# Attention and MoE in one stream: two slices side by side on TensorE, x moved to another PSUM bank, its scaling one step later

## What is computed

```python
scores = (q @ k.T) / sqrt(64)               # 2 batches, 8 heads, 576 tokens, head size 64
kth    = 32nd largest of each row of scores
attn   = softmax(where(scores >= kth, scores, -1e9))
x      = (attn @ v) as 1152 tokens x 512
h      = x @ w_in                           # 512 -> 2048
x2     = (h * sigmoid(h)) @ w_out           # 2048 -> 512
P      = exp(x2 @ w_gate - max); 8 rounds: rows to 1, columns to 144
out    = sum over 8 experts e of P[:, e] * (relu(x2 @ w1[e]) @ w2[e])
```

## Time and profile before

| | |
|---|---|
| Median of 3 runs | 1322.34 us (1320.54 to 1323.52) |
| The profiled execution | 1318.93 us, its span 1317.1 us |
| Busy over the span | TensorE 96%, VectorE 50%, ScalarE 35%, GpSimd 28% |
| Granted TensorE clock | 1.000 (mean over the span) |
| First stage | 0 to about 508 us |

### The profile page before, as it was taken

The page is one execution under the profiler, slowest core; times in us unless marked ns, Lnnn a source line. Parts: engine busy times, 40 slices in busy tenths (PEclk is TensorE's granted clock), DMA queues, the critical chain, the costliest instruction groups (busy, mean ns, idle before and its releaser), DMA issues.

```text
span 1317.1 us, 21296 instructions
## 1 busy us (share of the span) xinstructions
PE 1262.9 (96%) x8109; PEld 1117.0 (85%) x8109; DVE 664.9 (50%) x1485; ACT 456.9 (35%) x960; POOL 365.8 (28%) x321
## 2 busy tenths in 40 slices
PE   6888999999999999999999999999999999999999
PEld 4677787877777899898898898898898998998997
DVE  5999999999999326422222222222222222222222
ACT  3666766667667333021121121121120220220210
POOL 2665434434343422031131131130230230330300
PEclk9999999999999999999999999999999999999999
DMA  5863746636535542120120120110110110210001
GB/s 142 287 214 122 270 158 222 220 97 225 201 120 223 229 194 96 32 64 19 46 64 13 51 64 0 64 64 0 64 64 0 64 61 3 64 49 15 0 0 72
DMA packets 72929, 130.14 MB, mean 99 GB/s; under 512 B 42016, under 2 KB 42016, under 8 KB 63648
## 3 DMA queue, kind: packets, MB, share of 16 engines
q1 hardware_dynamic: 72864, 129.27, 28.6%
HBM read 110.12 MB, written 19.14 MB: 98 GB/s over the span
## 4 chain that ended last, share of the span: by engine, by line
PE 77%; DVE 13%; POOL 5%; ACT 3%; issue 2%; DMA 0%; SPq 0%; ACTq 0%
PE banks L409 24%; PE banks L411 23%; PE banks L410 23%; DVE stats L862 5%; DVE rest L873 5%; POOL probs L1110 2%; POOL wd_lo L1088 2%; PE banks L477 1%; POOL wu_lo L1088 1%; PE banks L444 1%; DVE g_f L926 1%; PE banks L453 1%; PE banks L470 1%; ACT scores L685 1%; ACT wu_hi L761 1%
## 5 line engine op out<-in xcount | busy, mean ns | idle before, releaser
L822 ACT ACTIVATE h_hi<-banks 128x384 fp32r<-128x384 f32 x192 | 94.5, 492 | 624.5 <-PE banks L411 624.5
L409 PE MATMUL banks<-x_lo,wu_hi 128*128 128x384 f32 x768 | 257.3, 335 | 0.0
L411 PE MATMUL banks<-x_hi,wu_hi 128*128 128x384 f32 x768 | 256.8, 334 | 0.0
L410 PE MATMUL banks<-x_hi,wu_lo 128*128 128x384 f32 x768 | 256.6, 334 | 0.0
L1088 POOL TENSOR_TENSOR wu_lo<-wu_raw,wu_hi 128x512 fp32r<-128x512 f32 x76 | 95.8, 1288 | 559.2 <-ACT wu_hi L761 552.3
L987 DVE SCALAR_TENSOR_TENSOR h_lo<-banks,h_hi 128x384 fp32r<-128x384 f32 x192 | 106.7, 557 | 281.7 <-ACT h_hi L822 281.7
L1029 DVE SCALAR_TENSOR_TENSOR y_acc<-banks,plan_e,y_acc 128x512 f32<-128x512 f32 x135 | 101.4, 751 | 272.3 <-PE banks L411 272.3
L409 PE MATMUL banks<-wd_lo,h_hi 128*128 128x512 f32 x576 | 227.2, 394 | 0.0
L411 PE MATMUL banks<-wd_hi,h_hi 128*128 128x512 f32 x576 | 227.0, 394 | 0.0
L410 PE MATMUL banks<-wd_hi,h_lo 128*128 128x512 f32 x576 | 227.0, 394 | 0.0
L862 DVE MAX8 stats<-rest 128x8 f32<-128x576 f32 x216 | 155.9, 748 | 0.1
(11 more groups left out here) (104 smaller groups left out, 1805.1 us busy)
## 6 DMA issues: line engine op xcount, KB each, us to landing
wu_raw<-in_moe_w_dram SPq DMA_DIRECT2D x32, 512.0 KB, 3.7
wd_raw<-in_moe_w_dram SPq DMA_DIRECT2D x32, 512.0 KB, 3.7
wu_hi<-kept_up_hi SPq DMA_DIRECT2D x14, 1024.0 KB, 5.9
wu_lo<-kept_up_lo SPq DMA_DIRECT2D x14, 1024.0 KB, 8.7
wd_hi<-kept_down_hi SPq DMA_DIRECT2D x14, 1024.0 KB, 6.0
wd_lo<-kept_down_lo SPq DMA_DIRECT2D x14, 1024.0 KB, 8.6
q_nat<-in_q_dram SPq DMA_DIRECT2D x64, 72.0 KB, 2.2
wu_raw<-in_moe_w_in_dram SPq DMA_DIRECT2D x8, 512.0 KB, 4.9
```

The costliest lines, as they stand in the source:

```text
L409: pe.matmul(to, a_hi, b_lo, start=first, stop=False)
L410: pe.matmul(to, a_lo, b_hi, start=False, stop=False)
L411: return pe.matmul(to, a_hi, b_hi, start=False, stop=last)
L822: act.activation(h_hi[:, f, CH * c:CH * (c + 1)], ps_up[:, at % UBANKS, 0:CH], ACT.Relu).then_inc(h_hi_done, 1)
```

## The change

- TensorE's step is reordered. Before: slice 0, weigh values, scores, spread, slice 1, transposes of probabilities, transposes of a head. After: scores, spread (of the tile one step older), slice 0, slice 1, weigh values, transposes of probabilities, transposes of a head.
- x of a unit moves from the second bank of `ps_t` to the bank of K transposed. `transpose_probs` no longer waits for its copy; `weigh_values` waits for the copies of K and Q, and the transposes of K wait for the copied x.
- The sums are spread and x is scaled one step later; their reciprocals get a second pair of columns.
- `least_kept` scales its two columns with two one-input `tensor_scalar` instead of one two-input `tensor_tensor` with a constant tile.
- The slices begin 5 steps behind the attention instead of 4, and everything tied to them shifts by one step. `keep_clock` gives 12 products a step instead of 10.
- ScalarE copies scores earlier in its step, and both split pieces come ahead of the penalty.

```diff
-FIRST_SLICE = 4
+FIRST_SLICE = 5
-STEPS = range(ALL + NT + 5)
+STEPS = range(ALL + NT + 6)
-        XO, RO = P, QT
+        XO, RO = QT, QT
+        def reciprocal_of(tile):
+            at = 36 + tile // 2 % 2
+            return stats[:, tile % 2, at:at + 1]
...
-            def transpose_head(hh, spread):
+            def transpose_head(hh, spread, weighed):
...
                 need(pe, x_scaled, spread)
                 if hh // H % 2 == 0:
+                    need(pe, o_copied, weighed)
...
             def transpose_probs(tile):
...
-                need(pe, o_copied, units_by(tile - 1))
...
             def weigh_values(tile):
...
                 pe.wait_ge(pT_copied, tile + 1)
+                pe.wait_ge(kq_ready, heads_by(tile + 4))
...
-                            last = pe.matmul(ps_t[D * j:D * (j + 1), 1, XO:XO + P],
+                            last = pe.matmul(ps_kq[D * j:D * (j + 1), 0, XO:XO + P],
...
             def spread_sums(tile):
...
-                pe.wait_ge(kq_ready, heads_by(tile + 4))
+                pe.wait_ge(kq_ready, heads_by(tile + 5))
...
             for step in STEPS:
+                if step + 1 < ALL:
+                    scores_of(step + 1)
+                if 0 <= step - 4 < ALL:
+                    spread_sums(step - 4)
                 silu_slice(slice_at(step, 0))
                 if step < NT + FIRST_SLICE:
-                    keep_clock(ps_m[:, 1, 0:P], 4)
-                if 0 <= step - 3 < ALL:
-                    weigh_values(step - 3)
-                if step + 1 < ALL:
-                    scores_of(step + 1)
-                if 0 <= step - 3 < ALL:
-                    spread_sums(step - 3)
+                    keep_clock(ps_m[:, 1, 0:P], 6)
...
                 silu_slice(slice_at(step, 1))
                 if step < NT + FIRST_SLICE:
                     keep_clock(ps_m[:, 1, 0:P], 6)
+                if 0 <= step - 3 < ALL:
+                    weigh_values(step - 3)
                 if 0 <= step - 2 < ALL:
                     transpose_probs(step - 2)
-                transpose_head(head_at(step + 2), units_by(step - 3))
+                transpose_head(head_at(step + 2), units_by(step - 4), units_by(step - 3))
```

ScalarE's step, where `copy_scores` and `copy_output` move:

```diff
                 if 0 <= step - 3 < ALL:
                     copy_pT(step - 3)
+                if step + 1 < ALL:
+                    copy_scores(step + 1)
                 g_high(slice_at(step - 1, 0))
...
                 g_high(slice_at(step - 1, 1))
-                if 0 <= step - 3 < ALL:
-                    copy_output(step - 3)
-                if step + 1 < ALL:
-                    copy_scores(step + 1)
                 split_pieces(pieces_at(step, 0))
+                split_pieces(pieces_at(step, 1))
                 if 0 <= step - 1 < ALL:
                     penalise(step - 1)
-                split_pieces(pieces_at(step, 1))
                 take_slice(slice_at(step, 1))
+                if 0 <= step - 3 < ALL:
+                    copy_output(step - 3)
                 copy_kq(head_at(step + 2))
```

VectorE's step, and the biases:

```diff
-                dve.tensor_tensor(st[:, 32:34], st[:, 0:TOPK:TOPK - 1], factors[:, :], ALU.mult).then_inc(kth_ready, 1)
+                dve.tensor_scalar(st[:, 32:33], st[:, 0:1], -(D ** -0.5), None, ALU.mult)
+                dve.tensor_scalar(st[:, 33:34], st[:, TOPK - 1:TOPK], PENALTY, None, ALU.mult).then_inc(kth_ready, 1)
...
                 if old:
                     search(step - 1, 2)
+                if 0 <= step - 3 < ALL:
+                    guard_sum(step - 3)
                 if new:
                     search(step, 0)
...
                 if old:
                     least_kept(step - 1)
+                if 0 <= step - 4 < ALL:
+                    scale_output(step - 4)
                 if new:
                     remove(step, 1)
                 take_slice(slice_at(step, 0))
-                if 0 <= step - 2 < ALL:
-                    guard_sum(step - 2)
-                if 0 <= step - 3 < ALL:
-                    scale_output(step - 3)
```

More of the change, by code:

```diff
@@ L500, in spread_sums @@
                         last = pe.matmul(ps_kq[D * j:D * (j + 1), 1, RO:RO + P],
-                                         stats[:, (tile - 1 + j) % 2, 35:36].to_broadcast([P, D]), ident[:, :],
+                                         reciprocal_of(tile - 1 + j).to_broadcast([P, D]), ident[:, :],
                                          start=True, stop=True)
@@ L791, in _ @@
                     copy_pT(step - 3)
+                if step + 1 < ALL:
+                    copy_scores(step + 1)
                 g_high(slice_at(step - 1, 0))
-                if step % NT == 3 and NT <= step < ALL + NT:
+                if step % NT == 4 and NT <= step < ALL + NT:
                     split_output(step // NT - 1, 2)
@@ L798, in _ @@
                 g_high(slice_at(step - 1, 1))
+                split_pieces(pieces_at(step, 0))
+                split_pieces(pieces_at(step, 1))
+                if 0 <= step - 1 < ALL:
+                    penalise(step - 1)
+                take_slice(slice_at(step, 1))
                 if 0 <= step - 3 < ALL:
                     copy_output(step - 3)
-                if step + 1 < ALL:
-                    copy_scores(step + 1)
-                split_pieces(pieces_at(step, 0))
-                if 0 <= step - 1 < ALL:
-                    penalise(step - 1)
-                split_pieces(pieces_at(step, 1))
-                take_slice(slice_at(step, 1))
                 copy_kq(head_at(step + 2))
-                if step % NT == 17 and step < ALL:
-                    split_output(step // NT, 0)
-                if step % NT == 6 and 2 * NT < step < ALL:
+                if step % NT == 0 and 0 < step < ALL + NT:
+                    split_output(step // NT - 1, 0)
+                if step % NT == 7 and 2 * NT < step < ALL:
                     sums_high(step // NT - 2)
@@ L886, in guard_sum @@
                 dve.wait_ge(exp_done, tile + 1)
-                dve.tensor_scalar(st[:, 36:37], st[:, 34:35], 1e-9, None, ALU.add).then_inc(guarded, 1)
+                dve.tensor_scalar(st[:, 35:36], st[:, 34:35], 1e-9, None, ALU.add).then_inc(guarded, 1)
             def invert_sum(tile):
@@ L891, in invert_sum @@
                 dve.wait_ge(guarded, tile + 1)
-                dve.reciprocal(st[:, 35:36], st[:, 36:37]).then_inc(rinv_ready, 1)
+                dve.reciprocal(reciprocal_of(tile), st[:, 35:36]).then_inc(rinv_ready, 1)
             def scale_output(tile):
@@ L947, in _ @@
                               ALU.subtract).then_inc(gate_split, 1)
-            dve.wait_ge(made, 6)
+            dve.wait_ge(made, 4)
             for step in STEPS:
@@ L978, in _ @@
                     split_pieces(pieces_at(step, 1))
-                if step == ALL + 6:
+                if step == ALL + 7:
                     split_sums(QUARTERS - 2, slice(0, KD))
@@ L1128, in _ @@
                     split_pieces(pieces_at(step, 1))
-                if step % NT == 0 and 0 < step < ALL + NT:
+                if step % NT == 1 and 1 < step < ALL + NT:
                     output_lows(step // NT - 1, 0)
-                if step % NT in (7, 8) and 2 * NT < step < ALL:
-                    sums_low(step // NT - 2, step % NT - 7)
+                if step % NT in (8, 9) and 2 * NT < step < ALL:
+                    sums_low(step // NT - 2, step % NT - 8)
             pool.wait_ge(lane_max, 1)
```

25 lines of the change are left out of this document (11 added, 14 removed).

## The result

The changed kernel takes 1338.5 us (median of 4 runs, 1337.2 to 1339.0) against 1322.3 us. The ratio is 1.0124 with a 95% interval of 1.0112 to 1.0136: slower by 16 us, where the prediction said 1322.5 us and at most 1334. The profiled execution has a span of 1335.4 us, 18.3 us more than before.

The account below looks back on a forecast made before the run. VectorE was taken nearly to set the pace of the attention steps, TensorE little behind; stretch sums of -2.7 us plus 3.2 for coupling gave +0.5 on the profiled 1318.9, which lies 3.4 under the median: 1322.5 us, range 1309 to 1334.

Parts of the forecast that it names:

- The one-input biases: VectorE's 32nd-score scaling: 12.7 us of excess from GpSimd's lock goes, the pair costs 1.4 us, net gain 11.3 us.
- rival (d): VectorE's scaling: one-input operations keep the lock, so that part does nothing: +2 to +3 us, 1325; chance 0.06.
- The head's stall: TensorE before scores: waits for ScalarE's copies of a head just transposed, 0.96 or 0.66 us each, 24.0 us for 30.
- rival (c): Head's copies come late on ScalarE, 1.72 us a head; TensorE bounds everywhere: +10 to +20 us, 1332 to 1342; chance 0.22.
- rival (b): Attention steps: VectorE is the only bound, TensorE's stalls fall into slack: -16.8 us, 1305.5, halfway 1314; chance 0.22.
- the sum as the greater of two ledgers: Attention stretches: each takes the longer of TensorE's and VectorE's work; the stretches and the tail sum to -2.7 us.
- The half of 6.5 us allowed for coupling: Three slice stretches: today they exceed the greater ledger by 6.5 us in all; 3.2 us added to the forecast.
- The early stretch: 22 to 118 us: TensorE 91.6, VectorE 83 of 96 us, so -4.4 us; with the five steps after it, -0.7.
- Fillers: TensorE, 23 steps ahead of the slices: 112 more filler instructions at 0.12 us, 13.4 us, 9 of them in the stretches.
- Slices later: End of attention: one step's slices, 1.78 at 1.59 us, move from under VectorE to behind it, +2.8 us.
- The pair's saving: TensorE: a second slice directly behind the first takes 1.59 instead of 1.77 us, 0.18 a pair, 2.5 us a quarter.

Follow-up runs that it names:

- a_early: Changed kernel with K and Q of a head transposed, copied and loaded one step earlier: 1324.2 us, ratio 1.002 to the kernel before.
- a_act: Changed kernel with ScalarE's copy of scores back behind the exponential and the high parts: 1335.4 us, ratio 1.0103 to the kernel before.
- a_early_act: Changed kernel with heads transposed one step earlier and ScalarE's copy of scores back behind the exponential: 1318.2 us, ratio 0.9968 to the kernel before.
- b_bias: Kernel before with only the two biases made by one-input operations: 1317.6 us, ratio 0.9966.
- b_late: Kernel before with only the slices and all tied to them one step later: 1316.5 us, ratio 0.996.
- a_early_act_ring: Changed kernel with heads one step earlier, scores' copy behind the high parts, and high parts of weights first on ScalarE: 1310.7 us, ratio 0.9918 to kernel before.
- b_all: Kernel before with one-input biases, high parts of weights ahead of the exponential, and slices one step later: 1304.8 us, ratio 0.9879.
- b_bias_ring: Kernel before with one-input biases and the high parts of both weight pieces ahead of the exponential on ScalarE: 1308.7 us, ratio 0.9895.
- a_fill10: Changed kernel with 10 filler products a step instead of 12 in the 23 steps ahead of the first slice: 1339.5 us, ratio 1.0139 to kernel before.
- a_two: Changed kernel with the two biases from one two-input operation again: 1342.3 us, ratio 1.0148 to the kernel before.
- a_ring_fill10: Changed kernel with high parts ahead of the scores' copy and the exponential, and 10 filler products a step: 1327.7 us, ratio 1.005 to kernel before.

## Why the prediction was wrong, step by step

**The one-input biases: right in size, wrong in effect.** The excess of 12.7 us went away in full, at no price for the pair (0.02 us a step was booked). The Trainium skill (SBUF, "Who interferes with whom") says that a one-input tensor_scalar can enter a two-port mode and contend with GpSimd as well, if its operands meet that mode's conditions. For one column nothing of it shows: 138 instructions in the groups above average 0.144 and 0.135 us; rival (d) is out. But 11.3 us on an engine is not 11.3 us at the end: undone or done alone it is 3.8 and 4.1 us. 7.7 of the 12.7 us (0.43 x 18) lay in the early steps, where the ring took them.

**The head's stall: right.** 24.0 us were booked for 30 heads, 25.4 measured, and ScalarE was prompt: the mean wait at scores is 14.2/23 = 0.62 us in the later quarters, as forecast (0.4 to 0.7). In the early stretch it is 6.4 us in 7 waits, 0.91 each, above the forecast but under the 1.1 us that would have meant rival (c). That rival had the right sign and its time range, 1332 to 1342, holds the result; its mechanism, late copies at 1.72 us a head, did not take place, so its hit is luck. (In rival (b), 18 steps at 5.2 us against 104.6 make -11.0 and not -10.7 us; nothing hangs on it.)

**The step that failed: the sum as the greater of two ledgers.** It let a stall on TensorE vanish wherever VectorE's ledger was as long. Quarter 2 shows it. TensorE's ledger there said 105.1 us, of which 7.7 were head stalls, 97.4 without. Read from start to start in the trace, the 18 steps take 111.3 us between transposes of P, 14.9 of them stalls, 96.4 without. The work and the head stalls (7.2) are as booked. Not booked are the other 7.7 us: 4.2 at the first slice behind scores (a slice starts 2.22 instead of 1.70 us before the next in the mean of 8, the low part's wait), 2.3 from the transposes of P to what follows (0.67 instead of 0.54 us), 1.2 in second slices (1.67 instead of the booked 1.59). With all of them TensorE's ledger is the greater one wherever slices run, VectorE's idle time is 31 us where 20 were forecast, and the greater part of each stall is paid: taking the heads' 25.4 us away gives 14.4 us, and behind tile 22's mark 11.2 of 16.0. It is not all of it, and the parts don't simply add: in quarter 2 the heads' 7.2 us give back 3.8 alone (a_early), the scores' copy alone gives nothing (112.1 us still, a_act), and the two together 7.4 (104.7 us, a_early_act). The half of 6.5 us allowed for coupling had no ground in a mechanism.

**A wait that was not listed.** The diff moves `copy_scores` ahead of the high parts. The prediction names the move and prices only ScalarE's promptness for K and Q. What the moved instruction itself waits for (GpSimd's subtraction), and what is then queued behind it, was not asked. TensorE's waits for low parts are 9.2 us from 118 to 440 us, before 2.4; moving the copy back takes 4.8 of them away, worth 3.1 us alone and 6.0 once the heads are out of the way. The other 4.4 us stay without the move. The longest of them (1.39 us, at 289.07 in a_act) is GpSimd's own queue: the high part is ready at 286.66, but GpSimd makes the low part of x from 285.37 (1.42 us) and then a subtraction (1.42 us), and starts on the slice's low part only at 288.12. The subtraction at 141.63 in the earlier trace rows held a hint: it had itself waited 3.66 us for ScalarE, so its end, for which the copy waits, could come late.

**The early stretch: a third bound.** Forecast -0.7 us, measured +0.9. Both ledgers (91.6 and 83 us for 96) were under the time that the stretch took, and 4.4 us were booked as gain. The gap was not slack but the ring of ScalarE and GpSimd at 5.95 us a step. The 93.3 busy us that made VectorE look like the bound held some 7 us of stretched multiplies: with them gone it is 86.45 us at the same pace (b_bias). The ring stood in the trace of before, in ScalarE's list of waits from 20 to 118 us, of which the prediction makes nothing:
```profile
ACT probs L697 <- POOL probs L1110: 31.5, 16, 2.7
```
16 waits in 16 steps, 2 us each, is what this ring looks like. In the changed kernel the same wait has another name, since the copy of scores now comes first (its list, same stretch):
```profile
ACT scores L690 <- POOL probs L1114: 26.8, 16, 2.9
```
The ring also takes rival (b) down: VectorE alone would have given 5.2 us a step there, and only kernels with the ring cut come near that pace.

**Fillers.** The extra products, booked at 13.4 us, were mostly covered by the ring: taken away alone they give nothing, taken away with the ring's cut the pair gives 10.9 us. How much of the 10.9 is theirs, no run tells apart; with heads early as well, 10 instead of 12 gives nothing.

**Slices later, and side by side.** The +2.8 us at the end measured +2.5 (b_late). That the same edit saves some 7 us in the steps (4.6 + 2.5) was missed, so in the old order its sign was wrong; in the new order it was not undone. The new order itself takes 883.3 us behind the transposes of tile 71, 4.1 more than before and 1.6 more than b_late, and a_early keeps that; where the 1.6 come from is open. The pair's saving is smaller than booked (1.67 instead of 1.59 us a second slice). With the heads' stall gone and the low parts' wait halved, the new order (a_early_act_ring, 1310.7 us) is 6 us above the old one with its own remedies (b_all, 1304.8 us). The marks of the two profiled executions (spans 1308.4 and 1304.6 us) say where. Tiles 4 to 22 take 96.0 against 93.8 us and the part behind tile 71 890.8 against 888.9, while quarter 2 takes 104.8 against 105.4 and tiles 54 to 71 95.3 against 96.0. So the new order has not paid over the whole, yet in these two stretches, where slices run in nearly every place, it is 0.6 and 0.7 us ahead. The loss lies mostly in the stretch with two fillers more a step and in the tail.

**The account.** From 1338.5 us: -14.4 heads early, -6.0 scores' copy back, -7.5 ring, together -27.8 = 1310.7 us. Still open: how b_late's gain in the steps divides over them (its profiled execution, with a span of 1317.6 us, was its slowest and shows little of it), and why the transposes of P start 0.67 us apart from what follows instead of 0.54.

## What to carry to other kernels

Before summing engines' busy times stretch by stretch, look through the waits of the engines that are not busy: a wait that occurs once in every step, at about the same length, can be a ring over in-order queues, which bounds the pace though neither of its engines is full. Moving one instruction of it ahead, as b_bias_ring does, is the test. When an instruction is moved forward in a queue, ask what it waits for and who stands behind it, not only what it costs. And where transposes, their copy and the product that reads it come in a row, put a step between them: here that was worth 14 us.

## What the runs showed of the hardware that was not expected

With ten products a step the granted TensorE clock is 1.00 over the early stretch in the kernel before, but not in every kernel of that order: b_bias, which changes nothing on TensorE, has 0.96 there, 0.91 up to 60 us and 1.00 behind. In the changed order, where the ten lie in one burst between scores and the rest, it stays low (a_fill10, table of stretches):
```profile
22.00:60.00 38.00, 31.40 (x259) 25.34 (x258) 36.71 (x99) 25.03 (x52) 24.88 (x20) 0.92 0.66 214
60.00:118.00 58.00, 51.59 (x449) 42.26 (x449) 49.43 (x137) 38.32 (x79) 35.14 (x28) 0.88 0.54 181
```
The changed kernel itself, with twelve, holds it:
```profile
60.00:118.00 58.00, 53.78 (x525) 44.93 (x523) 52.07 (x144) 39.09 (x80) 37.08 (x29) 1.00 0.60 186
```
Of the two levels the full one is 2.4 GHz; a mean of 0.88 means that TensorE spent part of the stretch at the lower one (1.2 GHz). But twelve products are no guarantee. a_early and a_early_act_ring hold 1.00 over the early stretch as well, a_act has 0.98, a_early_act 0.96, and so has a_two, each with twelve:
```profile
22.00:118.00 96.00, 87.04 (x784) 72.02 (x784) 93.34 (x219) 63.56 (x129) 61.37 (x48) 0.96 0.59 194
```
With ten the mean was 1.00, 0.98 (b_late, a_ring_fill10), 0.96, 0.95 and 0.90; the profile shows one execution of each kernel. The two lowest of them are kernels of the new order. These runs give no number of products that keeps the clock. Whether the burst or the longer gap elsewhere in the step brings it down, no run here tells apart.

The length of the old two-input multiply depended on what GpSimd was doing, up to 1.04 us, while a one-column operation with one input took 0.13 to 0.15 us under the same subtractions. The nine-column one-input operation of the earlier trace rows did stretch, to 0.90 us, so "one input" is not the whole rule; where between one column and nine it changes, no run here shows.
